# A three-part kernel on one core: where in its slot a chunk of the rational layer is divided

## The reference

```
x = attention(q, k, v)                      # 2 x 8 heads, 576 tokens, band of 32 (plain or dilated by 4)
for e in range(4):
    out += p[:, e:e+1] * (relu(x @ w1[e]) @ w2[e])
x = out
h = x @ w_in                                # 512 -> 2048
P = a[0] + a[1]*h + a[2]*h*h + a[3]*h*h*h
Q = 1.0 + abs(b[0])*abs(h) + abs(b[1])*h*h
g = P / (Q + 1e-6)
out = g @ w_out                             # 2048 -> 512
```

## Time and profile before

| what | value |
|---|---|
| median of 3 runs (range) | 683.92 us (682.25 to 684.38) |
| the profiled execution, its own time | 684.68 us |
| its span, first to last instruction | 682.9 us |
| TensorE matmul, busy | 655.4 us, 96% of the span |
| VectorE, ScalarE, GpSimd, busy | 45%, 44%, 32% |
| mean granted TensorE clock, share of full | 0.982 |
| chain of work that ended last | TensorE 91% of it |

### The profile page before, as it was taken

One profiled execution on the slowest core, in us unless ns is written; L12 is line 12 of the kernel. 1 busy time (PEld: TensorE's weight loads), 2 busy tenths in 40 slices (PEclk: granted clock), 3 DMA queues, 4 the chain that ended last, 5 costly groups with the idle time before them and its releaser, 6 DMA issues.

```text
span 682.9 us, 9783 instructions
## 1 busy us (share of the span) xinstructions
PE 655.4 (96%) x3716; PEld 586.3 (86%) x3716; DVE 307.8 (45%) x599; ACT 298.1 (44%) x756; POOL 217.4 (32%) x218
## 2 busy tenths in 40 slices
PE   4789999999999999999999999999999999999996
PEld 3678888999999999999999999998899999988884
DVE  6445555121121212121212122225888888888885
ACT  5677555222211122211222211235677777776663
POOL 4467222033310133310133300125542466632221
PEclk9589999999999999999999999999999999999999
DMA  9526410000320001420001320001310000001011
GB/s 312 209 93 209 138 48 1 1 1 31 124 93 1 0 1 35 129 84 1 0 1 62 123 62 1 0 1 62 123 62 1 0 2 1 1 1 47 0 47 47
DMA packets 13079, 36.83 MB, mean 54 GB/s; under 512 B 1832, under 2 KB 2856, under 8 KB 13032
## 3 DMA queue, kind: packets, MB, share of 16 engines
q1 hardware_dynamic: 13032, 36.20, 15.6%
HBM read 33.84 MB, written 2.36 MB: 53 GB/s over the span
## 4 chain that ended last, share of the span: by engine, by line
PE 91%; ACT 3%; DVE 2%; DMA 2%; issue 1%; POOL 0%; POOLq 0%; DVEq 0%; ACTq 0%
PE ps_h L376 44%; PE ps_o L393 42%; DMA scratch<-in_qk_plain 2%; PE ps_a L326 2%; ACT scratch L474 1%; PE ps_o L353 1%; PE ps_a L338 1%; PE ps_q L338 1%; DVE acc L706 0%; PE ps_b L353 0%; DVE scratch L643 0%; PE ps_a L416 0%; ACT scratch L581 0%; DVE scratch L786 0%; DVE scratch L776 0%
## 5 line engine op out<-in xcount | busy, mean ns | idle before, releaser
L376 PE MATMUL ps_h<-x_hi,w_hi 128*128 128x384 f32 (+1 forms) x608 | 202.9, 334 | 0.0
L376 PE MATMUL ps_h<-x_hi,w_lo 128*128 128x384 f32 (+1 forms) x608 | 200.8, 330 | 0.0
L376 PE MATMUL ps_h<-x_lo,w_hi 128*128 128x384 f32 (+1 forms) x608 | 200.1, 329 | 0.0
L691 DVE SCALAR_TENSOR_TENSOR h_lo<-ps_h,h_hi 128x384 fp32r<-128x384 f32 (+1 forms) x104 | 54.7, 526 | 272.4 <-ACT h_hi L497 272.4
L393 PE MATMUL ps_o<-w_hi,h_hi 128*128 128x512 f32 x432 | 169.9, 393 | 7.7 <-POOL h_lo L861 3.2
L497 ACT ACTIVATE h_hi<-ps_h 128x384 fp32r<-128x384 f32 (+1 forms) x104 | 48.6, 467 | 289.8 <-PE ps_h L376 289.7
L393 PE MATMUL ps_o<-w_hi,h_lo 128*128 128x512 f32 x432 | 170.8, 395 | 0.0
L393 PE MATMUL ps_o<-w_lo,h_hi 128*128 128x512 f32 x432 | 170.5, 395 | 0.0
L850 POOL TENSOR_TENSOR w_lo<-raw,w_hi 128x512 fp32r<-128x512 f32 x48 | 61.8, 1288 | 216.2 <-ACT w_hi L503 215.6
L376 PEld LDWEIGHTS ps_h<-x_hi,w_hi 128*128 128x128 f32 x608 | 115.7, 190 | 7.4 <-issue 0.3
L376 PEld LDWEIGHTS ps_h<-x_lo,w_hi 128*128 128x128 f32 x608 | 115.6, 190 | 5.6
(11 more groups left out here) (79 smaller groups left out, 574.6 us busy)
## 6 DMA issues: line engine op xcount, KB each, us to landing
raw<-in_weights SPq DMA_DIRECT2D x48, 512.0 KB, 3.6
scratch<-in_qk_dil SPq DMA_DIRECT2D x8, 352.0 KB, 4.6
scratch<-in_qk_plain SPq DMA_DIRECT2D x8, 304.0 KB, 5.9
out_t<-acc SPq DMA_DIRECT2D x9, 256.0 KB, 2.1
scratch<-in_v_dil SPq DMA_DIRECT2D x8, 208.0 KB
scratch<-in_v_plain SPq DMA_DIRECT2D x8, 192.0 KB, 4.9
prob<-in_probs SPq DMA_DIRECT2D x1, 18.0 KB, 13.0
a_sb<-in_a SPq DMA_DIRECT2D x1, 2.0 KB, 11.8
```

Of the source, the lines that this page charges most:

```text
L376: last = nc.tensor.matmul(h_of(k, f), w[:, f, dc, :], x, start=dc == 0 and i == 0, stop=dc == DC - 1 and i == 2)
L691: nc.vector.scalar_tensor_tensor(out=h_lo[:, s % RING, 0:n], in0=h_of(k, f), scalar=0.0, in1=h_hi[:, s % RING, 0:n].bitcast(F32), op0=ALU. ...
```

## The change

It moves steps of the rational slots, and changes no arithmetic but where it is done.

- ScalarE, slot c: `read_h(c)`, `guess(c)`, `keep_sums`, `high_rational(c-1)`, `high_x2`.
- VectorE, slot c: `from_h(c)`, `take_sums`, `divide(c)`, `low_x2`.
- GpSimd, slot c: the refills and then `low(c-1)`.
- The low part of the last chunk, c = 47, is made on VectorE.
- 1/Q goes into `ps_b` for all chunks of piece 13 (`ps_a` is there for the turned tiles) and into the two banks in turn from c = 8; the waits of `guess` and `turn_x2` follow that.

```diff
 def y_bank_of_chunk(c):
-    return (c if c < 4 else (1, 1)[c - 4] if c < 6 else c + 1) % 2
+    return 1 if c < FC else c % 2
@@ turn_x2
-                if 2 <= i < 6:
+                if 2 <= i <= 6:
                     pe.wait_ge(x2_lo, i - 1)
-                elif i == 6:
-                    pe.wait_ge(g_done, 3)
@@ guess
-                if c < 2:
-                    act.wait_ge(x2_lo, c + 5)
-                elif c < 4:
-                    act.wait_ge(g_done, c - 1)
-                elif c < 7:
+                if c == 0:
+                    act.wait_ge(x2_lo, 6)
+                elif c < FC:
                     act.wait_ge(g_done, c)
-                elif c == 7:
+                elif c == FC:
                     act.wait_ge(x2_lo, NT)
@@ scalar
                     read_h(k, f)
-                    if c >= 2:
-                        high_rational(c - 2)
-                    if c >= 1:
-                        guess(c - 1)
+                    guess(c)
+                    if f == LAG - 1 and expert_of(k - 1) == MOE:
+                        keep_sums(k - 1)
+                    if c:
+                        high_rational(c - 1)
                     if x2_slot(k, f) is not None:
                         high_x2(x2_slot(k, f))
-                    if f == LAG - 1 and expert_of(k - 1) == MOE:
-                        keep_sums(k - 1)
-            c = len(ITER) * FC - S0
-            high_rational(c - 2)
-            guess(c - 1)
-            high_rational(c - 1)
+            high_rational(len(ITER) * FC - S0 - 1)
@@ vector
                     from_h(k, f)
-                    if c:
-                        divide(c - 1)
+                    if f == LAG - 1 and expert_of(k - 1) != MOE:
+                        take_sums(k - 1)
+                    divide(c)
                     if x2_slot(k, f) is not None:
                         low_x2(x2_slot(k, f))
-                    if f == LAG - 1 and expert_of(k - 1) != MOE:
-                        take_sums(k - 1)
-            divide(len(ITER) * FC - S0 - 1)
+
+            c = len(ITER) * FC - S0 - 1
+            dve.wait_ge(hi_rational, c + 1)
+            dve.wait_ge(lo_rational, c)
+            nc.vector.tensor_tensor(h_lo[:, (S0 + c) % RING, :], h_full[:, c % SLOTS],
+                                    h_hi[:, (S0 + c) % RING, :].bitcast(F32), ALU.subtract).then_inc(lo_rational, 1)
             take_sums(len(ITER) - 1)
@@ gpsimd
-                    if c >= 2:
-                        low(c - 2)
                     if is_first(k):
                         high_w2(e, f)
                         low_w2(e, f)
                     if is_last(k) and e + 1 < EXPERTS:
                         high_w1(e + 1, f)
                         low_w1(e + 1, f)
-            c = len(ITER) * FC - S0
-            low(c - 2)
-            low(c - 1)
+                    if c:
+                        low(c - 1)
```

## The result

The changed kernel takes 674.05 us (median of 4 runs, 673.62 to 675.67) against 683.09 for the kernel before (4 runs): a ratio of 0.9875, 95% interval 0.985 to 0.9899, or 9.0 us less. Run once more on another chip it gave 0.9871 (0.9851 to 0.9891). The profiled execution took 675.67 us with a span of 673.9; the one of before took 684.68 with 682.9.

What follows compares the result with a forecast made beforehand. TensorE, busy 96% of the span, was taken as the bound, so only its waits could be won: sums 5.1 plus end 3.5, 8.6 us off, forecasting a median of 675.3 us, range 673.8 to 678.6.

Steps and rivals of the forecast that it cites:

- The three waits for sums: TensorE at c = 2, 34 and 42: with take_sums ahead of divide all three waits go, 5.1 us off.
- the 0.41 laid down: At c = 2: the sums free TensorE at 476.20, 0.41 us before it wants to start at 476.61.
- The end: Last chunks, 45 to 47: own-slot guess and divide leave one wait of about 0.4, 3.5 us off.
- Steady slots: Slots with nothing else in them: a loop of 3.6 us fits the slot of 4.19, so 0 us.
- The backlog after the sums: Slots behind VectorE's sums: next slot 1.2 late, the following one 0.6, then back in time.
- Refills, last low part, `keep_sums`: GpSimd's refills ahead of low parts, chunk 47's low part on VectorE, keep_sums at c = 10, 18, 26: 0 us.
- The sum: All terms together, in the rational slots: 5.1 + 3.5 = 8.6 us off.
- Sums late: Rival, sums: the three waits remain in part and only the end gains, 3.5 us, 680.4; chance 0.08.
- The end gaining less: Rival, end: chunk 46's high part queues behind guess(47), costing 1 us more, 676.3; chance 0.10.
- No difference at all: Rival: some wait put at zero binds and leaves times within 0.3% of before, 2 us; chance 0.03.
- The slower one: Rival: the ScalarE-VectorE loop outgrows the slot from 4.2 us, gain eaten at about 4.4, up to 694; chance 0.04.

Runs made afterwards that it cites:

- e1: The kernel before with one edit, take_sums put ahead of divide(c-1) on VectorE: 677.87 us, ratio 0.9932.
- e3: The changed kernel with take_sums put back behind divide(c) on VectorE: 678.48 us, ratio 0.9942 against the kernel before.
- e9: The kernel before with take_sums ahead of divide, and guess and divide in the chunk's own slot only from c = 43: 673.60 us, ratio 0.9864.
- e8: The changed kernel with GpSimd's low(c-1) put ahead of the slot's refills: 673.50 us, ratio 0.9875 against the kernel before.
- e2: The changed kernel with the last low part put back on GpSimd: 673.46 us, ratio 0.9859 against the kernel before.
- e5: The changed kernel with one more VectorE operation in each rational slot, into an unused tile: 677.90 us, ratio 0.993 against the kernel before.
- e6: The changed kernel with two more VectorE operations in each rational slot, into an unused tile: 706.01 us, ratio 1.0336 against the kernel before.
- e7: The changed kernel with 1/Q in SBUF instead of a PSUM bank: 695.73 us, ratio 1.0192 against the kernel before.

## Why the prediction was right

675.3 was forecast for the median and 674.05 came; in the range, 1.25 below, and only 0.25 above its low end. Of the 1.25, 0.83 is the base: the forecast started from a median of 683.92, and with a fourth run the kernel before has 683.09. As a difference, 8.6 was forecast and 9.0 measured.

- **The three waits for sums, 5.1**: 5.03 by the twins' starts, 4.93 by e1, 4.47 by e3. Right. The margin came out at the 0.41 laid down: 474.88 + 0.89 = 475.77 for an outer product at 476.18. The hand-over can be read in e3, where TensorE does wait: sums at 475.09, outer product at 475.99, 0.90.
- **The end, 3.5**: 668.47 - 661.70 = 6.77 from the first to the last of the four outer products, where it was 10.16 and a restart of 0.11: 3.50. Right to a hundredth, which is some luck, since the term is a difference of two chains of some ten steps; by the experiments, which take the change apart, it is 3.6 to 4.1.
- **Steady slots, 0**: slots stayed at 4.19, and L768 starts 0.70 after L762, 0.17 more than without a wait; I had about 0.1. Right, and e9 shows the same from the other side. The backlog after the sums went as laid out, a little smaller: the next slot's L757 stands at 613.66, where in undisturbed slots it would be 612.66 (608.47 + 4.19), 1.0 late where I had 1.2; the one behind it is 0.4 late (617.23 against 616.85) where I had 0.6, and the third is in time. The 0.2 are a misreading: I took 1.98 from the sums at c = 2, but those at c = 34 hold VectorE for 1.80 only (610.16 to 611.96).
- **Refills, last low part, `keep_sums`, 0**: e8 shows the first, e2 the second. `keep_sums` stays in its old place in e9, which has the gain all the same, and the twins' starts don't move at c = 10, 18 or 26.
- **The sum**: 8.6 was forecast for the rational slots, and the rational part fell by 8.56 and 8.61 in the two profiles. The other 0.4 of the 9.0 lies ahead of the first rational slot, in code that is the same (464.26 against 463.82). It is all there when the first inner product of the experts starts (L376, at 61.77 and 61.33), so it is scatter of the attention part.
- **The rivals.** Sums late: did not happen, and e3 gives its price, 4.5. The end gaining less: not so, each step of its chain came within 0.03. No difference at all: excluded by the interval, which ends at 0.9899. The slower one, that the loop outgrows the slot: not here, but e5, e6 and e7 show where it begins. I had it begin at a loop of 4.2 and eat the gain at 4.4. That was too kind. At 4.1 (e5) the rational part is already 4.7 longer than the changed kernel's, and at 4.4 to 4.6 (e7) 20.8, more than twice the gain, because I set the loop against the slot and left out the jobs of every eighth slot. With e5's loop the change would still have been a gain of 0.7%; the point where nothing is left lies between e5's loop and e7's. So the chance given to this rival rested on a sum that was too low, and the forecast was safe from it because the loop stayed at 3.6.

## What to carry to other kernels

Read the bound engine's waits by the job that ends them, not by the engine. Here six waits were two causes, a short job queued behind a long one (sums behind a division) and a pipeline spread over slots whose tail nothing covers, and each could be priced and taken away alone; the tighter order was needed only in the last five slots. When a chain over two engines is set against a slot, add to its length what the odd jobs cost, divided by the slots between them, since a spare of 0.1 a slot does not work off a job of 2 us in the eight slots to the next one.

## What was not expected of the hardware

- **A wait of 2 us can cost more than its length.** In e6 TensorE stands 2.94 us, and the matmuls behind it are slow (timeline):

```profile
593.29 0.77 PE L394 MATMUL ps_o<-w_hi,h_hi 128*128 128x512 f32 x1 [2.94 <-ACT acc L609]
593.85 0.63 PE L394 MATMUL ps_o<-w_lo,h_hi 128*128 128x512 f32 x1
594.28 0.63 PE L394 MATMUL ps_o<-w_hi,h_lo 128*128 128x512 f32 x1
```

  The granted clock, 1.00 ahead of the wait, stands at 0.50 in the first 2 us after it, the lower of the two levels (1.2 GHz). In steps of 0.43 instead of 0.23 TensorE loses 1.4 us before it is back at 1.00. The same fall to 0.50 stands behind the other long waits in the rational slots of e6 (1.84, 2.19, 2.95, 2.96, 2.93) and e7 (3.37, 2.49, 2.07, 2.24), at once or within 0.9 us of the restart. The shortest of them:

```profile
516.78 0.47 PE L394 MATMUL ps_o<-w_hi,h_hi 128*128 128x512 f32 x1 [1.84 <-ACT acc L609]
```

  No fall stands behind the waits of 1.0 to 1.5 in the kernel before, 1.32 in e7, 1.72 at the end of e5, or 2.24 at the end of e6, where the clock reads 1.00 throughout. So the length of the wait does not decide it alone: 2.24 us came out both ways. The waits in the kernel before cost only their length, the overlap of 0.17 and a restart of about 0.1.
- **An operation that is shut out looks busy.** In e7 VectorE's L772 reads 1.29 instead of 0.56, and no wait is shown.
